# Seven block products for eight in the gate and value products, on units of 1024 tokens

## What is computed

```python
qn = q / (norm(q, axis=1) + 1e-6); kn = k / (norm(k, axis=1) + 1e-6)
a = softmax(kn.transpose(0, 2, 1) @ qn / tau)          # 256 x 256 for each batch
x = (v @ a).reshape(12032, 256)
x = (sigmoid(x @ w_gate) * (x @ w_val)) @ w_out        # 1536 hidden channels
h = x @ w2_in; out = (h - tanh(h)) @ w2_out            # 2048 hidden channels
```

## Time and profile before

| | |
|---|---|
| time, median of 3 runs | 2296.06 us (2293.49 to 2296.17) |
| the profiled execution | 2294.44 us, of which the span from the first to the last instruction is 2292.6 us |
| instructions on PE | 12060 |
| busy: PE, DVE, ACT, POOL | 99%, 60%, 48%, 26% of the span |
| moved by DMA | 245.61 MB, 107 GB/s over the span |

### The profile page before, as it was taken

The page is one execution under the profiler, slowest core; times in us unless marked ns, Lnnn a source line. Parts: engine busy times, 40 slices in busy tenths (PEclk is TensorE's granted clock), DMA queues, the critical chain, the costliest instruction groups (busy, mean ns, idle before and its releaser), DMA issues.

```text
span 2292.6 us, 35724 instructions
## 1 busy us (share of the span) xinstructions
PE 2276.8 (99%) x12060; PEld 1976.5 (86%) x12060; DVE 1371.7 (60%) x2767; ACT 1092.0 (48%) x1968; POOL 604.2 (26%) x492
## 2 busy tenths in 40 slices
PE   8999999999999999999999999999999999999998
PEld 7888888888888888888998888888888888888898
DVE  6747656556566565565664755655646556556565
ACT  5645535445345354453453544534535435445354
POOL 3483213123032131230350311302203113023032
PEclk9999999999999999999999999999999999999999
DMA  9764232233142232322442323223223232233143
GB/s 332 222 220 139 67 90 97 76 112 104 50 137 73 82 103 75 111 97 53 154 133 58 108 82 105 96 61 126 89 66 126 68 98 96 66 121 100 44 138 104
DMA packets 240409, 245.61 MB, mean 107 GB/s; under 512 B 203360, under 2 KB 203616, under 8 KB 240352
## 3 DMA queue, kind: packets, MB, share of 16 engines
q1 hardware_dynamic: 234352, 225.29, 31.9%
q0 software_dynamic: 4400, 19.40, 2.4%
q10 hardware_dynamic: 1600, 0.20, 0.1%
HBM read 225.18 MB, written 19.66 MB: 107 GB/s over the span
## 4 chain that ended last, share of the span: by engine, by line
PE 95%; DMA 2%; DVE 2%; ACT 1%; issue 0%; SPq 0%; ACTq 0%; DVEq 0%
PE up L1189 56%; PE x_acc L1189 29%; PE acc L1189 10%; DMA qk_in<-in_k 2%; DVE sq_sum L845 1%; PE x_acc L1215 0%; ACT up L615 0%; DMA w_ring<-w_sums 0%; SPq L420 0%; DVE up L985 0%; DVE expd L862 0%; DVE val_w_lo L923 0%; DVE norm L875 0%; ACT func_out L671 0%; ACT g L699 0%
## 5 line engine op out<-in xcount | busy, mean ns | idle before, releaser
L578 POOL TENSOR_TENSOR g<-t_sums,g 128x512 fp32r<-128x512 f32 (+1 forms) x384 | 486.4, 1273 | 1587.0 <-ACT g L708 1587.0
L671 ACT ACTIVATE func_out<-up 128x512 f32<-128x512 f32 (+1 forms) x672 | 393.6, 588 | 650.2 <-PE up L1189 649.2
L957 DVE TENSOR_TENSOR up<-up,func_out 128x512 f32<-128x512 f32 (+1 forms) x288 | 197.5, 686 | 408.3 <-ACT func_out L671 408.2
L1189 PE MATMUL x_acc<-g,w_ring 128*128 128x256 f32 (+1 forms) x2304 | 306.2, 282 | 0.0
L961 DVE TENSOR_TENSOR g_lo<-up,g_hi 128x512 fp32r<-128x512 f32 (+1 forms) x288 | 195.9, 680 | 177.6 <-ACT g_hi L679 177.4
L1189 PE MATMUL up<-x_lo,in_w_hi 128*128 128x512 f32 (+1 forms) x768 | 299.0, 389 | 0.4 <-DVE x_lo L947 0.2
L1189 PE MATMUL up<-x_hi,in_w_lo 128*128 128x512 f32 (+1 forms) x768 | 296.9, 387 | 0.0
L1189 PE MATMUL up<-x_hi,in_w_hi 128*128 128x512 f32 (+1 forms) x768 | 295.6, 385 | 0.0
L708 ACT ACTIVATE g<-t_sums 128x512 fp32r<-128x512 f32 (+1 forms) x384 | 238.0, 620 | 108.0 <-DVE t_sums L1010 107.4
L1189 PEld LDWEIGHTS x_acc<-g,w_ring 128*128 128x128 f32 x2304 | 288.8, 192 | 0.0
L679 ACT ACTIVATE g_hi<-up 128x512 fp32r<-128x512 f32 (+1 forms) x288 | 169.6, 589 | 219.3 <-DVE up L957 219.1
(11 more groups left out here) (201 smaller groups left out, 3222.3 us busy)
## 6 DMA issues: line engine op xcount, KB each, us to landing
w_ring<-w_sums SPq DMA_DIRECT2D x192, 896.0 KB, 4.5
v_in<-in_v SPq DMA_DIRECT2D x176, 64.0 KB, 2.2
out_rows<-out_sb SPq DMA_DIRECT2D x176, 64.0 KB, 1.8
qk_in<-in_q SPq DMA_DIRECT2D x29, 384.0 KB, 4.0
qk_in<-in_k SPq DMA_DIRECT2D x29, 384.0 KB, 5.5
w_sums<-g POOLq DMA_DIRECT2D x4, 1792.0 KB, 7.6
w_stage<-in_moe_w_out POOLq DMA_DIRECT2D x4, 512.0 KB, 5.0
w_stage<-in_moe_w_gate POOLq DMA_DIRECT2D x3, 512.0 KB, 7.7
```

Source lines behind the costliest of these rows:

```text
L578: pool.tensor_tensor(lo[:, cut, 0:half], t_sums[:, first - T1:first - T1 + 2, 0:half], hi[:, cut, 0:half].bitcast(F32), ALU.subtract).then ...
L671: act.activation(func_out[:, half, cut], func_bank(kind, i, tile)[:, cut], ACT.Sigmoid if kind == "U" else ACT.Tanh).then_inc(func_made, 1)
L957: dve.tensor_tensor(bank_cut, bank_cut, func[:, cut], ALU.mult).then_inc(prod_made, 1)
L1189: mm = pe.matmul(psum, a, b, start=start and n == 0, stop=stop and n == 2, skip_group_check=shared_bank)
```

## The change

Work goes in units of 1024 tokens (two subs of W = 512; the last unit of each batch has two subs of 448). The first block's gate and value weights are no longer in SBUF. For each pair of hidden blocks and each of gate and value there is a record of 896 KB in DRAM (`u_records`: three blocks and four sums, high and low parts), and for each pair of `w_out` blocks one of 512 KB (`d_records`). Records of `u_records` and `w2_sums` come through one ring of four slots, `d_records` through one of two. The first unit is computed plainly, from folded weights still in SBUF, while the records for batch one are made and stored; the records of batch two are made from raw parts inside unit 1.

A gate or value block pair is now seven products of three matmuls. Four open the four `up` banks; ACT copies two banks out, DVE adds in PSUM, and the last products accumulate on those sums:

```diff
+    U_STEPS = {"M1": (A11, V11, A_), "M5": (S1, VT1, D_), "M6": (S2, VT2, B_), "M7": (S3, VT3, C_),
+               "M2": (A12, V21, A_), "M4": (A22, VT4, C_), "M3": (S4, V22, D_)}
...
+            def add_up(u_steps, copied, summed, n, w, other_summed, other_done):
...
+                dve.wait_ge(u_steps, PRODUCTS * n + M6)
+                dve.wait_ge(copied, 2 * n + 1)
...
+                dve.tensor_tensor(u2, up[B_][:, cut], held[:, HELD_A, cut], ALU.add
+                                  ).then_inc(summed, 1)
+                dve.wait_ge(u_steps, PRODUCTS * n + M7)
+                dve.wait_ge(summed, done + 1)
+                dve.tensor_tensor(up[C_][:, cut], up[C_][:, cut], u2, ALU.add).then_inc(summed, 1)
+                dve.wait_ge(copied, 2 * n + 2)
+                dve.wait_ge(summed, done + 2)
+                dve.tensor_tensor(up[B_][:, cut], up[C_][:, cut], held[:, HELD_D, cut], ALU.add
+                                  ).then_inc(summed, 1)
+                dve.tensor_tensor(up[D_][:, cut], up[D_][:, cut], u2, ALU.add).then_inc(summed, 1)
...
+            def opening_of_gate(t, p, w):
+                n, i = pair_no(t, p), G_OF[p]
+                loaded(t, i)
...
+                u_product(gate_steps, i, "M1", w)
...
+                u_product(gate_steps, i, "M5", w)
...
+                u_product(gate_steps, i, "M6", w)
+                u_product(gate_steps, i, "M7", w)
+                pe.wait_ge(gate_copied, 2 * n + 1)
+                u_product(gate_steps, i, "M2", w)
...
+            def end_of_gate(n, i, w):
+                pe.wait_ge(gate_summed, 4 * n + 3)
+                u_product(gate_steps, i, "M4", w)
+                pe.wait_ge(gate_summed, 4 * n + 4)
+                u_product(gate_steps, i, "M3", w)
...
+            def cycle(t, p, w):
+                opening_of_gate(t, p, w)
+                D(t, p - 1, 0, w)
+                end_of_gate(pair_no(t, p), G_OF[p], w)
+                D(t, p - 1, 1, w)
+                opening_of_val(t, p, w)
+                D(t, p - 1, 2, w)
+                end_of_val(t, p, w)
+                D(t, p - 1, 3, w)
```

The low halves of gate x value move from DVE to POOL. The second block takes both subs one after the other, 16 pairs k with `O(k-2)` behind P(k,0) and P(k,1). ACT copies the seven output sums out of PSUM (`copy_m`, in pair 9 for the first sub, at the start of the next unit for the second), POOL joins them after pair 10 and DVE turns the first sub after pair 12:

```diff
+        SUM_AT, TURN_AT = 10, 12
...
+            def both_subs(t, w, nxt):
+                for k in range(BOTH):
+                    lo_of_t(t, k, w)
...
+                    if k == SUM_AT:
+                        sum_out(t, 0, w)
...
+                    if k == TURN_AT:
+                        turn_out(t, 0, w)
```

SP issues all of this in one order:

```diff
+            def rest_of_tile(t, b, w, nxt, b_next, first=False):
+                for k in range(BOTH - 4):
+                    load_o(t, k, first)
+                    if k == 0 and not first:
+                        load_d(t, U_PAIRS - 1)
+                store(t, b, 0, w)
+                for k in range(BOTH - 4, BOTH - 1):
+                    load_o(t, k)
+                if nxt:
+                    sp.wait_ge(o_made, BOTH * t + O_OF.index(NEXT_G - SLOTS) + 1)
+                    load_ring(NEXT_G, u_records[b_next, record(0, 0)])
+                load_o(t, BOTH - 1)
```

The second batch's folding, in unit 1 between its first pair and the rest, and the first unit's sums:

```diff
+            def fold_again(t, n):
+                pe.wait_ge(raw_loaded[n], 32)
...
+                else:
+                    pe.wait_ge(whole_made, KC * (n - 1))
...
+            def hi_of_fold(n):
...
+                if n >= 2:
+                    act.wait_ge(fold_stored[n - 2], 32)
...
+                    for m in range(FOLDS):
+                        hi_of_fold(m)
...
+                        if m:
+                            hi_of_fold_sums(m - 1)
+                    hi_of_fold_sums(FOLDS - 1)
+                    act.wait_ge(fold_a_lo_made, 2 * FOLDS)
+                    act.wait_ge(fold_s_lo_made, FOLDS)
+                    hold_gate(n + 1, w)
...
+            def hi_of_u_sums(n):
+                if n:
+                    act.wait_ge(u_s_stored[n - 1], 32)
```

More of the change, by code:

```diff
@@ L76, in attn_two_mlp_kernel @@
     out_rows = out
[L81 to L146, removed]
+    ALL = slice(None)
@@ L187, in attn_two_mlp_kernel @@
         sums = expd
[L188 to L196, removed]
+        func_out = sb("func_out", [P, 4, W])
+        with ExitStack() as between_u:
+            m_copy_a = sb("m_copy_a", [P, 4 * W], F32, between_u)
@@ L224, in comb_rows, with pair_part, blocks_of_rows @@
+        def pair_part(k, part):
+            return parts_of(g2[k % G2_SLOTS], part)
+        def blocks_of_rows(rows):
+            first, second = (row.rearrange("p (r i c) -> p r i c", r=2, i=2) for row in rows)
+            return first[:, :, 0], second[:, :, 0], first[:, :, 1], second[:, :, 1]
         def comb_rows(q):
@@ new lines, in sums_and_lo_of_pair @@
+            def sums_and_lo_of_pair(t, k, w, first=False, fold=False):
+                half, n = w // 2, 2 * (BOTH * t + k)
+                hi, lo = pair_part(k, HI), pair_part(k, LO)
+                t1, t2, t3, t4 = (t_sums[:, m, 0:half] for m in range(4))
+                g11 = up[P_BANKS[2 * k % 4]][:, 0:half]
+                odd = up[P_BANKS[(2 * k + 1) % 4]]
+                g21, g22 = odd[:, 0:half], odd[:, half:w]
+                g12 = kept[:, 0:half]
+                done = 4 * (BOTH * t + k)
+                dve.wait_ge(p_hi_made, n + 1)
+                if not (first and k == 0):
+                    dve.wait_ge(t_lo_made, 2 * (BOTH * t + k))
+                if fold and k == 0:
+                    dve.wait_ge(fold_s_lo_made, FOLDS)
@@ L1157, in _ @@
             for n in range(EARLY_FOLDS):
[L1158 removed]
+                split_fold(n)
             make_sums(1)
[L1161 to L1170 removed]
@@ new lines, in _ @@
+            both_subs(0, W, W, first=True)
+            body(1, W, W, W, fold=True)
+            with dve.Fori(2, TILES_BATCH - 2) as t:
+                body(t, W, W, W)
+            body(TILES_BATCH - 2, W, W, W_END)
+            body(TILES_BATCH - 1, W_END, W, W)
+            body(TILES_BATCH, W, W_END, W)
+            with dve.Fori(TILES_BATCH + 1, TILES - 2) as t:
+                body(t, W, W, W)
+            body(TILES - 2, W, W, W_END)
+            body(TILES - 1, W_END, W, None)
+            turn_out(TILES - 1, 1, W_END)
@@ new lines, in down @@
+            def down(j, s, blk, w, first, last, frees=()):
+                weights = [d_ring[:, j // 2 % 2, :].rearrange("p (a c f) -> p a c f", a=2, c=2
+                                                              )[:, part, j % 2] for part in (HI, LO)]
+                for h in range(KC):
+                    if frees:
+                        pe.wait_ge(m_copied, frees[h])
+                    mm = product3(x2_banks[s][h][:, 0:w], both(weights, ALL, cols(h)),
+                                  both(G1, ALL, blk, slice(0, w)), first, last)
+                    if last and h == 0:
+                        mm.then_inc(x2_half_made, 1)
+                mm.then_inc(down_made, 1)
```

1727 lines of the change are left out of this document (1062 added, 665 removed).

## The result

The changed kernel takes **2490.6 us** (median of 4 runs, 2487.5 to 2492.9) against 2294.9 (median of 4, 2293.5 to 2296.2): ratio 1.0852, 95% interval [1.0833, 1.0871]. I forecast slower, 2381 us, and a range up to 2425: the direction was right, and the size lies 110 us above the forecast and 66 above the range.

The account below looks back on a forecast made before the run. PE was taken as the bound, its matmuls issued back to back. 2292.6 - 87.7 - 6 + 9 + 82 + 44 + 17 + 4.5 + 24 = 2379.4, with 1.8 outside the span 2381 us; range 2290 to 2425.

Parts of the forecast that it names:

- matmuls removed: First-block gate and value products: 252 matmuls per unit instead of 288, first unit plain; -87.7 us.
- waits at the change of batches: Between the two batches: 6 us taken as PE waits, rewritten by the change; -6 us.
- ring load behind the stores: Out weight 12 queued behind eight stores, so PE stalls before O(12): 6.8 us per unit (3.8 to 7.6), +82.
- folding: Second batch's records made in unit 1, rounds of about 11.5 us keep PE waiting; +44 us, bounds 36 to 50.
- first unit: ACT waits for stores of weight sums, late for sigmoids in every second chunk; +17 us, bounds 8 to 25.
- small waits: Three places per unit without a down block as cover, 0.25 to 0.3 us each; +9 us.
- the end: After the last matmul: ACT copies, POOL sums, DVE turns, stores go out, 10.1 us; +4.5 us.
- the clock: PE at half clock after gaps of 5 us or more: 1.6 us for each of 15; +24, bounds 0 to 60.
- rival that hid the ring load: Out weight 12 lands before O(12), no ring or clock term: 2275 us; chance 0.14.
- the one that kept the clock: The waits are there but PE's clock holds: 2357 us; chance 0.15.
- the one of lower bounds alone: Ring 46, folding 36, first unit 8, no clock term: 2304 us; chance 0.12.
- rival of slow additions: DVE's additions between products too slow, each half cycle stalls 0.3 us: 2421 us; chance 0.12.

Follow-up runs that it names:

- g1: Kernel before, with PE made to wait for four small POOL additions in each of 21 tiles; 2373.0 us, ratio 1.0346.
- e1: Changed kernel, with the first half's eight stores issued after out weights 12, 13 and 14 instead of ahead of them; 2385.0 us, ratio 1.0404.
- e2: Changed kernel, with ACT's four copies of the first half's output sums moved one step earlier in its queue; 2471.8 us, ratio 1.0783.
- e5: e4, with v loads issued after the folding and each fold's sums' high half made ahead of the next fold; 2315.2 us, ratio 1.0089.
- e4: Changed kernel with the edits of e1, e2 and e3 together; 2334.1 us, ratio 1.0174.
- e3: Changed kernel, with the two loops over units written out as single units on all five engines; 2461.8 us, ratio 1.0726.
- g2: Kernel before, with PE made to wait for eight small POOL additions in each of 21 tiles; 2423.6 us, ratio 1.0564.

## Why the prediction came out as it did

Each term, as forecast and as the changed kernel's trace has it:

| term | forecast | measured |
|---|---|---|
| matmuls removed | -87.7 | 396 fewer, as forecast |
| waits at the change of batches | -6 | 0 |
| ring load behind the stores | +82 | +75.8 |
| copies ahead of O(8) | 0 | +30.4 |
| loop returns | 0 | +16.6 |
| folding | +44 | +35.3 |
| first unit | +17 | +22.9 |
| small waits | +9 | +25.6 |
| the end | +4.5 | +6.0 |
| the clock | +24 | +71.5 |
| sum | +86.8 | +196.4 (the span: +196.8) |

*First unit* is 15.3 for sigmas with 3.1, 3.0 and 1.5 for down weights, the transpose and a low half. *Folding* is 13.4 + 7.3 + 5.1 + 9.5. *Small waits* are 3.3 for POOL's low half, 2.2 for DVE (L1384) and 20.1 that no view shows as idle: busy time grew by 91.6 against the forecast work (2280.7 - 2276.8 + 87.7), and 71.5 of it is clock. *The end* is 11.7 us behind the last matmul where the kernel before has 5.7.

**The clock: the step that failed most, 47.5 of the 110 us.** The sentence is "If it stays low as long as it took to fall, half of 3.2 us is lost: 1.6 for each of 15 gaps". Both factors were too small. A low stretch lasts 3.4 or 6.8 us (up to 13.7 around the longest gaps), 2.2 lost on average; and there are 33 of them: nine at O(8) and three at the loop returns, of which I had none, and nine in the first unit and the folding instead of three. The gaps at O(8) and the loops make 23.4 of the 47.5, the first unit and the folding 16.2 (21.0 for 4.8), the ring 7.8 (27.0 for 19.2). Counted with its clock, then, the stall at O(8) is 47.5 us of the miss and the loop returns are 22.9. The upper bound of 60 does not follow from its own words: a pair of 5.26 us at half speed costs 5.26 more, which at 15 gaps is 79. That is more than twice the 2.2 measured for a gap.

**Copies ahead of O(8), 30.4.** The sentence that failed is "plus 0.4 for ACT's four copies in pair 9": I followed the copies to POOL's sums and not to PE, whose O(8) waits for the same semaphore. The wait in `o_products` was in the code. I asked who is late behind the copies, and not who needs the banks.

**Loop returns, 16.6.** No step of mine had them, and nothing in the trace before pointed there. Why such a return costs so much stays open.

**The change of batches, 6.** The six microseconds were never waits. In the kernel before, the stretch from 1069.05 to 1252.13 is

```profile
1069.05:1252.13 183.08, 182.74 (x1037) 1.00 0.36 109
```

PE busy for 182.74 of 183.08. I had subtracted an estimate (69.8 for a tile of 384 tokens) and called the rest a wait without looking at the stretch. It is 2.8 short: the starts of 384-column matmuls lie 0.173 us apart and those of 192 columns 0.111, and 312 x 0.173 + 168 x 0.111 = 72.6. The other 3 us are four small transposing matmuls and delays of at most 0.34 us each.

**Small waits, 16.6 too few.** The three uncovered places are there (3.3 us at one of them). The 20.1 us without an idle row, 1.7 a unit, belong for the most part to the listed waits. A matmul of 512 columns is recorded as 0.39 us long while the next starts after 0.227, so each listed wait leaves out some 0.16 us: around the loop return above the starts lie 6.24 us apart, 6.01 more than usual, and the row says 5.85. From 100 us on the changed kernel has 94 waits, the smallest ones counted too, which leave out 15.7 us in all; the kernel before has 11 and 1.8. g1 agrees: 45.6 + 27.2 + 21 x 0.16 = 76.2, and its span is 76.1 longer.

**Right.** The rival that hid the ring load, the one that kept the clock and the one of lower bounds alone are all false. The ring stall: place, count and cause, shown by e1. That its size fits (6.3 a unit for 6.8) is partly luck: I had PE unhindered up to O(12), and the stall at O(8) hid a part of it. With that one cut down (e2) the ring stalls 7.8 us a unit, above my upper bound of 7.6. The additions between the products: first-block cycles take 15.0 to 15.1 us against the 14.96 forecast, and no wait for an addition is in the list, so the rival of slow additions is false. The first unit's waits for stores and the end are right in kind, 5.9 and 1.5 us too small. **Folding** had a fair size for partly the wrong reason: the first round waited 11.5 us for raw parts, which I had not priced, and e5 took 16.1 of e4's 34.5 us out with the stores left as they were.

The forecast's direction did not hang on the failed steps: without the clock, the copies and the loops the changed kernel would be near 2372 (2490.6 - 71.5 - 30.4 - 16.6), and still slower.

## What to carry to other kernels

Price a stall as its length plus what the clock takes behind it, and look first for stalls of 2 to 4 us, which cost 1.6 to 1.7 times their length here (2.2 us cost 3.7, 3.0 cost 4.8 and 3.8 cost 6.1), while gaps of up to 2.0 us in the changed kernel cost their length alone. On a queue that carries loads with a due time and stores without one, write the stores behind the last load that is due. Follow each added copy to everyone who waits for its semaphore, and check every "rest" of a subtraction in the stretch itself before it is called a wait. Here the seven products are worth 8.2 us a unit, and repairing the stalls around them brought the kernel from 2491 to 2300 us, still 0.3% above the kernel before.

## What the runs showed of the hardware

- A gap of 2.2 us in PE's stream was followed by a fall of the granted clock to half in 16 of 21 cases (g1), one of 3.0 to 3.3 us before O(8) in nine of ten (changed kernel), eight of ten (e1) and ten of ten (e3), one of 3.8 us in 21 of 21 (g2). The low stretch lasted 3.4 us, or 6.8 (ten of 21 in g2). Gaps of 1.1 us (e4) left the clock at 1.00.
- The fall came 2.5 to 3.7 us after PE stopped in g1, with PE already back at work.
- A loop's return cost PE 5.3 to 5.9 us in a body of one unit (3 of 3; 5.1 to 5.9 in e1), and nothing in the kernel before's body of one tile.
- In the folding, with 400 to 430 GB/s moving, raw parts of 512 KB landed 9.2 and 11.1 us after their issue (medians, 340 to 372 us); those issued from 372 to 380 us, where 178 GB/s moved on average, after 4.6 and 5.5.
